# Splitting the down-sampled keys as 112 and 32 instead of 128 and 16, in an attention kernel followed by two MLPs

## The reference, cut to what matters

```python
q_d = q.reshape(B, H, Sd, factor, D).mean(axis=3)      # Sd = 144, factor = 4; the same for k_d and v_d
out_up = np.repeat(sm_attn(q_d, k_d, v_d), factor, axis=2)
mask = np.abs(pos[:, None] - pos[None, :]) < factor
...                                                     # softmax over the masked scores, times v
x = attn_out.transpose(0, 2, 1, 3).reshape(B * S, H * D)   # 2304 x 512
h = x @ w_in;  x = (h - np.tanh(h)) @ w_out
gate = 1.0 / (1.0 + np.exp(-(x @ w_gate)))
return gate * (x @ w_val) @ w_out2
```

## Time and profile before

| | us |
|---|---|
| median of 3 runs | 898.12 (897.77 to 899.66) |
| the profiled execution's own time | 898.21 |
| its span, first to last instruction | 896.4 |
| PE busy (share of the span) | 881.3 (98%) |
| DVE busy | 580.5 (65%) |
| ACT busy | 381.2 (43%) |
| POOL busy | 286.6 (32%) |

### The profile page before, as it was taken

One profiled execution on the slowest core, in us unless ns is written; L12 is line 12 of the kernel. 1 busy time (PEld: TensorE's weight loads), 2 busy tenths in 40 slices (PEclk: granted clock), 3 DMA queues, 4 the chain that ended last, 5 costly groups with the idle time before them and its releaser, 6 DMA issues.

```text
span 896.4 us, 15665 instructions
## 1 busy us (share of the span) xinstructions
PE 881.3 (98%) x6088; PEld 829.9 (93%) x6088; DVE 580.5 (65%) x922; ACT 381.2 (43%) x720; POOL 286.6 (32%) x237
## 2 busy tenths in 40 slices
PE   7998999999999999999999999999999999999998
PEld 5877899999999999999999999999999999999997
DVE  8999876578756668565679656576444466444445
ACT  4777855455333344233354544453222243222221
POOL 5889776591030001030136558513100001000000
PEclk9999999999999999999999999999999999999999
DMA  8875497669554545455315777788755555755511
GB/s 259 248 232 159 178 350 275 239 228 403 186 207 171 212 141 213 168 187 201 118 48 209 283 282 282 281 337 320 281 212 211 212 211 211 262 231 211 211 48 70
DMA packets 36137, 197.01 MB, mean 220 GB/s; under 512 B 3712, under 2 KB 5248, under 8 KB 23008
## 3 DMA queue, kind: packets, MB, share of 16 engines
q1 hardware_dynamic: 29584, 162.16, 48.6%
q0 software_dynamic: 4032, 29.36, 8.7%
q10 hardware_dynamic: 2448, 4.49, 1.7%
HBM read 139.90 MB, written 56.10 MB: 219 GB/s over the span
## 4 chain that ended last, share of the span: by engine, by line
PE 92%; POOL 4%; DVE 2%; issue 1%; ACT 1%; DMA 0%; ACTq 0%; POOLq 0%; DVEq 0%
PE banks L848 48%; PE banks L920 22%; PE banks L1036 17%; PE banks L822 1%; PE banks L794 1%; POOL prob L589 1%; PE banks L779 1%; POOL v_four L582 1%; PE banks L768 1%; PE banks L839 1%; PE banks L811 1%; POOL win L629 0%; POOL prob_d L589 0%; POOL v_down L586 0%; DMA qk<-in_k_dram 0%
## 5 line engine op out<-in xcount | busy, mean ns | idle before, releaser
L848 PE MATMUL banks<-x_op,pair 128*128 128x384 f32 x1512 | 276.1, 335 | 0.0
L848 PEld LDWEIGHTS banks<-x_op,pair 128*128 128x128 f32 x1512 | 265.2, 188 | 7.2
L920 PE MATMUL banks<-g_parts,mid 128*128 128x384 f32 x1152 | 226.3, 335 | 1.4 <-DVE x_all L1498 1.3
L920 PEld LDWEIGHTS banks<-g_parts,mid 128*128 128x128 f32 x1152 | 201.7, 188 | 3.1 <-DVE x_all L1498 3.1
L848 PE MATMUL banks<-x_op,win 128*128 128x384 f32 x1008 | 201.4, 335 | 0.0
L848 PEld LDWEIGHTS banks<-x_op,win 128*128 128x128 f32 x1008 | 176.7, 188 | 0.8 <-issue 0.7
L1036 PE MATMUL banks<-wout,p_parts 128*128 128x512 f32 x648 | 162.9, 393 | 0.0
L1498 DVE TENSOR_TENSOR x_all<-banks,x_all 128x384 f32<-128x384 f32 x168 | 92.8, 555 | 83.8 <-PE banks L920 83.3
L1036 PEld LDWEIGHTS banks<-wout,p_parts 128*128 128x128 f32 x648 | 120.4, 188 | 20.7
L1624 DVE TENSOR_TENSOR x_all<-banks,x_all 128x512 f32<-128x512 f32 x90 | 62.1, 690 | 112.3 <-PE banks L1036 112.3
L648 POOL DMA_DIRECT2D wout<-kept_out x12 | 6.4, 537 | 211.4 <-PE banks L1036 211.4
(11 more groups left out here) (98 smaller groups left out, 985.5 us busy)
## 6 DMA issues: line engine op xcount, KB each, us to landing
pair<-kept_pair SPq DMA_DIRECT2D x24, 1792.0 KB, 10.5
win<-kept_in SPq DMA_DIRECT2D x16, 1792.0 KB, 7.5
kept_pair<-pair SPq DMA_DIRECT2D x12, 1792.0 KB, 11.7
mid<-kept_mid POOLq DMA_DIRECT2D x16, 1024.0 KB, 5.1
kept_in<-win SPq DMA_DIRECT2D x8, 1792.0 KB, 7.2
wout<-kept_out POOLq DMA_DIRECT2D x12, 1024.0 KB, 11.6
kept_mid<-mid SPq DMA_DIRECT2D x8, 1024.0 KB, 5.1
kept_out<-wout SPq DMA_DIRECT2D x6, 1024.0 KB, 15.0
```

Source lines behind the costliest of these rows:

```text
L848: mm = pe.matmul(bk[:, 0:T], weights[:, w, p - 1, kk, :], x_op[:, p - 1, x, kk, :], start=(first and kk == 0 and a == 0), stop=(last and k ...
L920: mm = pe.matmul(bk[:, 0:T], w[:, wp, f, m * P:(m + 1) * P], g[:, gp, 2 * f + t, :], start=(f == 0 and a == 0), stop=(f == 1 and a == 2))
```

## The change

The 144 down-sampled rows are split as 112 (`MOST`) and 32 (`FEW`). `v_four` loses its second half, so a unit's own additions on POOL run over 112 partitions and 256, then 128 elements. The 32 last rows of four units are loaded together into `v_few`, one tile of 128 partitions with unit `u` in partitions `32 * (u % 4)` onward, and added by `few_sums(k)`: two POOL additions (256 and 128 elements) for four units, in periods 1 and 2 whole, and split over periods 5 and 6, 9 and 13. There are four such loads instead of sixteen; each waits on SP for the sums before it. `down_values` waits for these sums as well. `turn_rest` turns 112 columns for the first part, and for the second 32, 64, 96 or 128 columns, so that the 32 rows lie at the partitions where the unit's values are.

Moved: `weight_sums(0)` from periods 5 and 6 to 3 and 4, its load split in two and issued at units 1 and 2 instead of at 2; `half_weight_high(0)` from 7 and 8 to 5 and 6; `first_weight_low`, two pieces each in 8 and 9, to one piece each in 6 to 9; the load of the second quad's weights split over units 9 and 10 instead of at 8; `weight_sums(1)` from 13 and 14 to 14 and 15; `half_weight_high(1, 0)` from period 15 to period 16 ahead of its other half; on DVE, `x_low` of products 1 and 7 in periods 13 and 14 from behind `local_sum(t)` to ahead of it. The two clearings of `v_four` on DVE, and SP's wait for them, go.

```diff
-    FEW = SD - P
-    KEYS = (slice(0, P), slice(SD - FEW - D, SD))
-    ROWS = (slice(0, P), slice(D, D + FEW))
+    FEW = P // 4
+    MOST = SD - FEW
...
+        def rows_of(u, c):
+            return slice(0, MOST) if c == 0 else slice(u % 4 * FEW, u % 4 * FEW + FEW)
...
-            def load_v_few(u):
-                wait(sp, s_vd, u - 1)
-                sp.dma_start(v_four[u % 2][ROWS[1], 1, :, :]...
+            def load_v_few(k):
+                wait(sp, s_few, 2 * k)
+                sp.dma_start(v_few[:, :, :].rearrange("p f n -> p (f n)"),
+                             bass.AP(v_flat.tensor, ..., [[P * S, 4], [FACTOR * P, FEW], [1, FACTOR * P]])).then_inc(s_vfew, 16)
...
-            sp.wait_ge(s_four, 2)
-            load_v_few(0)
             for u in range(UNITS):
-                if u + 1 < UNITS:
-                    load_v_few(u + 1)
                 if u + 3 < UNITS:
                     load_qk(u + 3)
                 load_v(u)
-                if u == 2:
-                    load_raw(0)
-                if u == 8:
-                    load_raw(1)
+                if u in (0, 1, 3, 7):
+                    load_v_few((0, 1, 3, 7).index(u))
+                if 1 <= u < 3:
+                    load_first_raw(0, u - 1)
+                if 9 <= u < 11:
+                    load_first_raw(1, u - 9)
...
-                pool.tensor_tensor(four[:, :, 0:2, :], four[:, :, 0:2, :], four[:, :, 2:4, :], ALU.add).then_inc(s_vd_step, 1)
+                pool.tensor_tensor(four[:, 0:2, :], four[:, 0:2, :], four[:, 2:4, :], ALU.add).then_inc(s_vd_step, 1)
...
-                pool.tensor_tensor(v_down[u % 2][:, :, :], four[:, :, 0, :], four[:, :, 1, :], ALU.add).then_inc(s_vd, 1)
+                pool.tensor_tensor(v_down[u % 2][:, :], four[:, 0, :], four[:, 1, :], ALU.add).then_inc(s_vd, 1)
+            def few_pairs(k):
+                pool.wait_ge(s_vfew, 16 * (k + 1))
+                pool.tensor_tensor(v_few[:, 0:2, :], v_few[:, 0:2, :], v_few[:, 2:4, :], ALU.add).then_inc(s_few, 1)
+            def few_fours(k):
+                wait(pool, s_vald, 4 * (k - 1))
+                pool.wait_ge(s_few, 2 * k + 1)
+                pool.tensor_tensor(v_few_down[k % 2][:, :], v_few[:, 0, :], v_few[:, 1, :], ALU.add).then_inc(s_few, 1)
...
                 if t < UNITS:
                     value_sums(t)
+                if t < 3:
+                    few_sums(t - 1)
+                if 3 <= t < 5:
+                    weight_sums(0, ((0, 1), (2, 3))[t - 3])
                 if t == 5:
-                    weight_sums(0, (0, 1))
+                    few_pairs(2)
+                if 6 <= t < 10:
+                    first_weight_low(t - 6)
                 if t == 6:
-                    weight_sums(0, (2, 3))
-                if t == 8:
-                    first_weight_low(0)
-                    first_weight_low(1)
+                    few_fours(2)
                 if t == 9:
-                    first_weight_low(2)
-                    first_weight_low(3)
+                    few_pairs(3)
                 if 10 <= t < 13:
                     x_sums(0, (t - 10,))
                 if t == 13:
-                    weight_sums(1, (0, 1))
-                if t == 14:
-                    weight_sums(1, (2, 3))
+                    few_fours(3)
+                if 14 <= t < 16:
+                    weight_sums(1, ((0, 1), (2, 3))[t - 14])
...
             def down_values(u):
                 pe.wait_ge(s_vd, u + 1)
+                pe.wait_ge(s_few, 2 * (u // 4 + 1))
...
-                if 7 <= t < 9:
-                    half_weight_high(0, t - 7)
+                if 5 <= t < 7:
+                    half_weight_high(0, t - 5)
...
-                if t == 15:
-                    half_weight_high(1, 0)
...
                 if t == UNITS:
+                    half_weight_high(1, 0)
                     half_weight_high(1, 1)
                     copy_c(0, C22)
                     copy_c(0, C21)
...
+                if 13 <= t < 15:
+                    x_low(0, (1, 7)[t - 13])
                 if t < UNITS:
                     local_sum(t)
-                if 13 <= t < 15:
-                    x_low(0, (1, 7)[t - 13])
```

More of the change, by code:

```diff
@@ L191, in attention_and_mlps @@
         early = Room(RING + 2 * WIN_BYTES, RING + 2 * WIN_BYTES + 4 * WS)
-        v_four = [room.tile(f"v_four{i}", [P, 2, FACTOR, P]) for i, room in enumerate((low, early))]
-        v_down = [low.tile(f"v_down{i}", [P, 2, P]) for i in range(2)]
+        v_four = [room.tile(f"v_four{i}", [MOST, FACTOR, P]) for i, room in enumerate((low, early))]
+        v_down = [low.tile(f"v_down{i}", [MOST, P]) for i in range(2)]
+        v_few = low.tile("v_few", [P, FACTOR, P])
+        v_few_down = [low.tile(f"v_few_down{i}", [P, P]) for i in range(2)]
         prob_d = [room.tile(f"prob_d{i}", [DROWS, 3, SD]) for i, room in enumerate((low, low, early))]
@@ L223, in attention_and_mlps @@
         s_zeros = sem("zeros_ready")
-        s_four = sem("v_four_cleared")
+        s_vfew = sem("v_few_loaded")
+        s_few = sem("v_few_sums")
         s_band = sem("band_ready")
@@ L421, in kept_mid_ready, with load_first_raw @@
                 sp.wait_ge(s_keptm[n % 3], 16 * (n // 3 + 1))
+            def load_first_raw(n, c):
+                sp.dma_start(win_raw[n][:, 2 * c:2 * c + 2, :].rearrange("p k n -> p (k n)"), w_in[n + c * Q1]).then_inc(s_raw[n], 16)
             def load_raw(n):
@@ L579, in value_sums, with few_sums @@
             def value_sums(u):
-                pool.wait_ge(s_v4[u % 2], 32 * (u // 2 + 1))
+                pool.wait_ge(s_v4[u % 2], 16 * (u // 2 + 1))
                 four = v_four[u % 2]
-                pool.tensor_tensor(four[:, :, 0:2, :], four[:, :, 0:2, :], four[:, :, 2:4, :], ALU.add).then_inc(s_vd_step, 1)
+                pool.tensor_tensor(four[:, 0:2, :], four[:, 0:2, :], four[:, 2:4, :], ALU.add).then_inc(s_vd_step, 1)
                 wait(pool, s_vald, u - 1)
                 pool.wait_ge(s_vd_step, u + 1)
-                pool.tensor_tensor(v_down[u % 2][:, :, :], four[:, :, 0, :], four[:, :, 1, :], ALU.add).then_inc(s_vd, 1)
+                pool.tensor_tensor(v_down[u % 2][:, :], four[:, 0, :], four[:, 1, :], ALU.add).then_inc(s_vd, 1)
+            def few_sums(k):
+                few_pairs(k)
+                few_fours(k)
+            def few_pairs(k):
[5 more added lines that the diff above has]
+                pool.tensor_tensor(v_few_down[k % 2][:, :], v_few[:, 0, :], v_few[:, 1, :], ALU.add).then_inc(s_few, 1)
             def scale_rows(view, inv, n, width):
@@ L600, in weight_sums @@
                 if su < Q1:
-                    pool.wait_ge(s_raw[su % 3], 16 * (su // 3 + 1))
+                    pool.wait_ge(s_raw[su % 3], raws(su))
                 else:
@@ L627, in first_weight_low @@
                 part = slice(piece * WS // 4, (piece + 1) * WS // 4)
-                pool.wait_ge(s_whi, highs(0))
+                pool.wait_ge(s_whi, highs(0) - 1 if piece < 2 else highs(0))
                 pool.tensor_tensor(dst[:, 1, :, :, :].rearrange("p o k n -> p (o k n)")[:, part], raw[:, :, :].rearrange("p o n -> p (o n)")[:, part],
@@ L807, in turn_rest @@
                 pe.transpose(bk[0:HALF, 0:HALF], prob[u % 3][0:HALF, first:first + HALF], ident[0:HALF, 0:HALF])
+                keys = slice(0, MOST) if hh == 0 else slice(SD - rows_of(u, 1).stop, SD)
                 for c in range(3):
                     spot = HALF + c * DROWS
-                    mm = pe.transpose(bk[0:ROWS[hh].stop, spot:spot + DROWS], prob_d[u % 3][:, c, KEYS[hh]],
-                                      ident[0:DROWS, 0:DROWS])
+                    mm = pe.transpose(bk[0:rows_of(u, hh).stop, spot:spot + DROWS], prob_d[u % 3][:, c, keys], ident[0:DROWS, 0:DROWS])
                 mm.then_inc(s_tr, 1)
@@ L1102, in copy_rest @@
                 wait(act, s_vald, u - 1)
-                rows = slice(0, ROWS[hh].stop)
+                rows = slice(0, max(HALF, rows_of(u, hh).stop))
                 act.activation(prob_tr[u % 2][rows, hh, :], bank[B_R[hh]][rows, 0:REST], ACT.Copy).then_inc(s_cr, 1)
@@ L1417, in _ @@
             dve.memset(zeros_b[:, :], 0.0).then_inc(s_zeros, 1)
-            for i in range(2):
-                dve.memset(v_four[i][:, 1, :, :], 0.0).then_inc(s_four, 1)
             for i in range(3):
```

14 lines of the change are left out of this document (8 added, 6 removed).

## The result

The changed kernel takes 904.11 us (median of 5 runs, 903.16 to 907.71), the kernel before beside it 899.48 (897.77 to 899.95): ratio 1.0064, 95% interval 1.0052 to 1.0076. The prediction said 893.8 and faster. The profiled execution took 903.76 with a span of 902.0, 5.6 above that of before (896.4).

A forecast was written before the change was run, and what follows sets the result against it. POOL was taken to bound the attention's second half, leaving PE 5.4 us idle to win. Unit 14 starts 5.15 us earlier (0.45 given back to DVE's lag), less ACT's 0.8, so 4.35 saved: 893.8 us, range 892.2 to 896.2.

The forecast's parts named there:

- what bounds the second half: Attention's second seven periods: POOL bounds them at 6.18 us each; after the change PE sets periods 3 to 15, at 5.46.
- POOL's prices: POOL's additions for a unit: 0.70 us for 256 elements, 0.43 for 128; `value_sums` 1.27, 0.83 less per unit.
- the seven waits of the earlier trace: In the kernel before, `turn_local` on PE waits seven times for POOL's `prob`, 5.1 us; predicted to go.
- B: Rival, `turn_rest` on PE: narrow turned columns are done as two passes, 2.3 us more, 896.1; chance 0.08.
- D: Rival, PE's period: 32-row products no longer run in pairs, narrow turns add 2.3; 7.6 us in all, 901.4; chance 0.03.
- ACT's 0.83 in period 16: `half_weight_high(1, 0)` moved ahead of `copy_c(0, .)` on ACT adds 0.83 us; product 5 on PE comes 0.8 later.
- A: Rival, before product 5: ACT's added 0.83 us in period 16 is absorbed, giving 893.0; chance 0.10.
- the few-load that is issued at 16.0: Units 4 to 7's load on SP: lands at about 20, POOL asks at 19.5; 0.5 us out of a 1.8 reserve.
- Rival C: Units 4 to 7's few-load takes 7.3 us, lands at 23.3 and holds POOL: +1.5, 895.3; decides past 21.8; chance 0.10.
- The lock of `x_low`: DVE's `x_low` in periods 13 and 14 waits for POOL's instruction: costs some 0.1 and 0.4 us, not 1.4.
- DVE's reserve: DVE's lag of 2.1 us at most after period 14 has reserves of 1.8 (POOL) and 1.3 (ACT); 0.45 taken back via `copy_local(14)`.
- The range: Whole kernel: 892.2 to 896.2 us, taking in A below, B to its price above, and the sum's bounds.

The follow-up runs named there:

- experiment 7: Two kernels on its base: first quad's weights two periods later, 899.09 us; then also units 4 to 7's few-load at unit 2, 897.62. Its table lists eleven traces' stops.
- experiment 1: Changed kernel with each few-load issued as four loads of 32 rows: 899.16 us, ratio 1.0008 to the kernel before.
- experiment 3: Changed kernel with four 32-row loads per few-load, and `x_low` of products 1 and 7 moved behind `write_x`: 897.42 us, ratio 0.9999 to the kernel before.
- experiment 7's base: Changed kernel with four 32-row loads per few-load, two `v_few` tiles, `x_low` behind `write_x`, `copy_c(0, .)` ahead of `half_weight_high(1, .)`: 897.61 us, ratio 0.9978 to the kernel before.

## Why the prediction was wrong, point by point

- **Right: what bounds the second half, and POOL's prices.** 112x256 takes 0.73 (said 0.70), 112x128 0.46 (0.43); from unit 2 to 12 PE sets 5.45 us a period, and the seven waits of the earlier trace rows are gone.
- **Right: B and D fall.** The turns take 0.45 for three in 32, 64, 96, 112 and 128 columns alike, the value products of a unit 0.64 in the chain where they took 0.66. PE's timeline of the changed kernel:

```profile
45.81 0.45 PE L841 MATMUL banks<-ident,prob_d 112*32 112x112 f32 x3
...
51.27 0.45 PE L841 MATMUL banks<-ident,prob_d 112*64 112x112 f32 x3
```

- **Right: ACT's 0.83 in period 16.** Product 5 waits 0.80 for `copy_c`; A falls.
- **The step that failed first: the few-load that is issued at 16.0 and lands at about 20, since "a 256 KB load took 4.0".** That row was of `v_four`, 256 KB too, but with 128 at the outside of its source. I priced by bytes what goes also by the shape of the source. Measured: issued at 18.40, 2.4 later, behind a first few-load that was late as well (POOL waits 1.6 us for it); 8.33 to landing, 4.3 more; landed at 26.73. With 32 rows outermost it takes 4.9, issued at 16.48. That would have been in time, but it isn't 4.0 either, and the first one still takes 7.7 amid the other loads. Rival C had the mechanism and its point of decision right, its size wrong (landing 23.3 and +1.5, measured 26.73 and +5.65) and its chance too low: "at half the bytes" was the same error.
- **The lock of `x_low`: "0.1 and 0.4, not 1.4".** Measured 1.42 and 2.42 against 0.95 undisturbed, so 0.5 and 1.5, and PE waits 1.48 for `write_x`. I reckoned with the end of one POOL instruction; it is the end of the unbroken run that counts. The rows of before fit this: `x_low` of 83.05 ended 0.8 behind the first of two POOL instructions, and between those two lay 0.14 us; I read it as the rule for any two, gap or not. And DVE's reserve was spent not through `copy_local` but through `write_x`, which I hadn't named among those behind `x_low`.
- **Not priced at all: what PE does after it has stood idle.** 3.42 us of idle cost 2.2 more, 1.48 cost 1.7 (1.85 and 2.22 for what takes 1.04 and 1.30), with the granted clock at 0.50. The terms for waits of that length were too small by this. It isn't a fixed charge: the waits of up to 1.0 in the kernel before left the clock at 1.00, and so did stops of 0.71, 0.72, 1.13 and 1.36 in the table of experiment 7, while 1.25 in experiment 1 and 1.44, 1.69 and 2.00 in that table brought it to 0.50.
- **The range** added small bounds to the forecast and left out the sizes that C and the lock really had. Its lower end, 892.2, is under every term named; the sum's own is 892.7. With the load right and `x_low` moved the kernel reaches 897.4, not 893.8: the gain from the periods is there (unit 1 to 12 at 5.45 each), but the first period gives back 3.2 us, unit 0 to 1 in 8.67 in experiment 3, which no rival held. That PE stops there is shown, why it does is not.

The best variants, 897.14 to 897.61, are about 0.2% under the kernel before, the edge of what can be told; of these only experiment 7's base has an interval (0.9969 to 0.9987) wholly below 1 by more than a tenth of a per cent.

## What to carry to other kernels

Price a transfer by the shape of its access pattern and by what else is in flight, not by its bytes alone: a load gathered over 4 far places with the 4 outermost took 8.33 us where the same bytes as four loads took 4.9, but only 8.53 against 7.7 where other loads filled the engines. When a median landing time is read from a list of issues, ask how many issues make up the whole. A VectorE instruction that reads two SBUF operands belongs where GpSimd is waiting, and last before DVE's own wait, not ahead of something that others wait for. When an edit takes the slack out of periods, price the idle time that it may bring to TensorE with the slower clock that may follow: nothing for the waits of up to 1.0 us in the kernel before, 1.7 for 1.48, 2.2 for 3.42.

## What the runs showed of the hardware that I had not expected

- 256 KB in 15.1, 8.53 and 7.7 us (the first few-load) and in 10.5, 8.33 and 4.9 us (the second) by an outermost source dimension of 2, 4 and 32; with 2 and nothing else in flight, 50 to 52 GB/s at a DMA share of 0.13 to 0.14.
- DVE's two-operand `x_low` (0.95 alone) was held until POOL made a gap: 2.42 and 2.43 us beside a run of POOL instructions with no gap between them, ending 0.8 us behind the run both times.
- In 3.42 us of idle time the granted clock fell to 0.50, where it stood for 6 us (28 to 34); PE's eight turns took 1.89 instead of 1.07. Stops of 1.13 and 1.36 us elsewhere left it at 1.00, waits of 1.25 and 1.48 did not.
- PE can stop for 0.7 to 2.0 us in the middle of a group with nothing that the trace names as releaser; it was absent in one execution in which a 256 KB load was issued one unit later. Its length goes with how late a 16 KB packet of the trace's instruction queue comes; what it waited for stays open.
